# A chunked recurrence: decays counted from a chunk's first token, a first solve level on eight tiles, and one product merged into another block

## The reference

```python
for t in range(S):
    y[:, :, t] = einsum('bhd,bhde->bhe', r_t, state)
    Sa = einsum('bhde,bhe->bhd', state, a_t)
    state = state * w_t[:, :, None, :] - einsum('bhd,bhe->bhde', Sa, b_t) \
            + einsum('bhd,bhe->bhde', v_t, k_t)
```

## Time and profile before

| | us |
|---|---|
| median of the runs | 992.89 |
| the profiled execution | 993.9 |
| its span | 992.2 |
| recurrence, start to the loop's second pass | 0 to 69.1 |
| recurrence, passes 1 to 22 of the loop | 69.1 to 384.4 |
| the two later layers | 384.4 to 992.2 |

### The profile page before, as it was taken

How to read it: one execution, slowest core, us unless ns; L and a number is a source line. 1 busy time by engine, 2 the same in 40 slices (tenths; PEclk the granted TensorE clock), 3 DMA queues, 4 the chain that set the end, 5 groups by cost and what they waited for, 6 DMA issues and landing times.

```text
span 992.2 us, 51897 instructions
## 1 busy us (share of the span) xinstructions
PE 947.2 (95%) x23581; PEld 732.5 (74%) x23582; DVE 465.9 (47%) x964; ACT 270.5 (27%) x503; POOL 275.8 (28%) x297
## 2 busy tenths in 40 slices
PE   4689999999999999999999999999999999999995
PEld 3579989899898996454554554557888888888884
DVE  5447877887887762423143143162352322222220
ACT  1224444444444442201202202202212122122120
POOL 4535566556656651000011010010052101111111
PEclk9789999999999999999999999999999999999999
DMA  5216442333333321780100100047421111001000
GB/s 147 64 50 209 140 123 89 114 104 119 96 115 111 89 72 41 238 271 0 38 27 24 42 28 20 1 133 256 130 88 61 34 34 39 23 28 33 27 29 3
DMA packets 57704, 81.63 MB, mean 82 GB/s; under 512 B 22274, under 2 KB 37454, under 8 KB 57648
## 3 DMA queue, kind: packets, MB, share of 16 engines
q1 hardware_dynamic: 33536, 58.87, 19.0%
q10 hardware_dynamic: 21088, 13.32, 5.2%
q0 software_dynamic: 3024, 8.72, 2.4%
HBM read 68.04 MB, written 14.45 MB: 83 GB/s over the span
## 4 chain that ended last, share of the span: by engine, by line
PE 91%; issue 3%; DVE 2%; DMA 2%; POOL 1%; ACTq 0%; ACT 0%; POOLq 0%; SPq 0%; DVEq 0%
PE ps_D L1478 14%; PE ps_D L224 12%; PE ps_G L1460 6%; PE ps_E L1460 6%; PE ps_B L236 5%; PE ps_E L956 5%; PE ps_B L188 3%; PE ps_G L1467 3%; PE ps_D L1039 3%; PE ps_A L930 3%; PE ps_G L188 3%; PE ps_D L990 2%; PE ps_E L954 2%; PE ps_E L188 2%; PE ps_D L930 2%
## 5 line engine op out<-in xcount | busy, mean ns | idle before, releaser
L1478 PE MATMUL ps_D<-room,hT 128*128 x496 | 139.1, 433 | 0.8 <-issue 0.8
L224 PE MATMUL ps_D<-room 128*128 128x384 f32 x384 | 126.7, 489 | 0.6 <-DVE room L291 0.6
L1478 PEld LDWEIGHTS ps_D<-room,hT 128*128 128x128 f32 x496 | 91.8, 190 | 35.9 <-issue 1.3
L224 PEld LDWEIGHTS ps_D<-room 128*128 128x128 f32 x384 | 72.1, 190 | 51.5 <-issue 1.6
L1421 POOL DMA_INDIRECT out<-y,token x31 | 35.6, 1147 | 258.3 <-DVE y L1585 224.7
L550 POOL DMA_INDIRECT sorted_rows<-rows,slot x24 | 23.9, 997 | 278.3 <-DVE slot L542 272.2
L894 POOL TENSOR_TENSOR room<-room 32x256 f32<-32x256 f32 x96 | 69.5, 724 | 106.5 <-DVE room L1310 101.1
L1521 ACT ACTIVATE hT<-ps_G 128x512 f32<-128x512 f32 x31 | 18.5, 598 | 217.6 <-PE ps_E L1467 211.4
L1585 DVE TENSOR_SCALAR y<-ps_D,x_in 128x320 f32<-128x320 f32 x31 | 17.0, 550 | 125.9 <-PE ps_D L1478 117.5
L1568 DVE COPY w_own<-room 128x1024 f32 x62 | 44.9, 729 | 62.3 <-PE ps_G L1460 33.8
L291 DVE TENSOR_TENSOR room<-ps_D,room 128x384 f32<-128x384 f32 x32 | 17.8, 558 | 113.2 <-PE ps_D L224 107.8
(11 more groups left out here) (225 smaller groups left out, 1646.2 us busy)
## 6 DMA issues: line engine op xcount, KB each, us to landing
room<-in_moe_w SPq DMA_DIRECT2D x8, 1280.0 KB, 12.6
room<-in_moe_w SPq DMA_DIRECT2D x8, 1024.0 KB, 9.2
room<-in_kb SPq DMA_DIRECT2D x48, 160.0 KB
room<-in_vt SPq DMA_DIRECT2D x24, 320.0 KB, 3.1
x_in<-sorted_rows ACTq DMA_DIRECT2D x27, 161.0 KB, 2.3
room<-in_w SPq DMA_DIRECT2D x48, 82.7 KB
room<-in_a SPq DMA_DIRECT2D x48, 80.0 KB
room<-in_r SPq DMA_DIRECT2D x48, 80.0 KB
```

The source lines that it names most:

```text
L224: mm = pe.matmul(self.vs_bank[n % 2][:, 0:TH], self.v[:, s, d * P:(d + 1) * P], self.wspT[:, s, t * TH:(t + 1) * TH], start=(s == 0), stop ...
L1478: mm = pe.matmul(self.ps_y, side.hT[:, u % 2, f, :], self.weights.w2[:, bass.ds(e, 1), f, :], start=(f == 0), stop=(f == self.NF - 1))
```

## The change

It does these things.

- All decays are counted from the first token. The backward scan, `grow`, the copy of the chunk's product and the 16-element reciprocal go. The forward products stay in a ring of four (`decay`), and one reciprocal of all 16 x 32 of them (`inverse`) takes their place; it stands between sum 2 and the mask on `scores_r`, and waits for `kb_start` of the chunk before. GpSimd makes `kb_start` (keys by `inverse`), then `a_start`, then the decayed `state`.
- Level 0 runs on eight tiles with 64 moving columns (the scores and a unit matrix), so that it gives both halves; VectorE adds the unit matrix (`summed(x, 0)`), in place of GpSimd. From there the systems stand on other quarters (`solved`), and the levels write two PSUM banks. `unknowns` runs on eight tiles.
- `own_part` is no block any more. Its 64 matmuls stand alternately with those of level 3, write `ps_A`, and `right_state` adds onto them in PSUM. VectorE's sum for the right-hand side becomes a copy on ScalarE, at the end of its step. Level 3 waits in addition for ScalarE's copy of `turn_kb`.
- `turn_kb` moves ahead of `scores_r`. VectorE's state sum moves ahead of the forward scan. ScalarE's copies of turned data take 40 of 64 columns.

```diff
 # TensorE's loop
-                    own_part(t)
+                    turn_kb(t)
                     scores_r(t)
                     doubling(t, 3)
-                    turn_kb(t)
                     scores_a(t)
 # own part, now inside doubling(t, 3)
+                def until_own(t):
+                    pe.wait_ge(ld_v, t.after16)
+                    pe.wait_ge(kn_d, t.later)
+
+                def own_part(mp, o, n, j):
+                    k = quad(2 * mp + 1 - o)
+                    return pe.matmul(A[solved(mp, o, j), j, n * HD:(n + 1) * HD], xa[k, o, n, j, :], v_tok[k, o, j, n, :],
+                                     start=(n == 0), stop=True, skip_group_check=True)
 # doubling
-                        if l == 1:
-                            pe.wait_ge(init_d, t.after4)
+                        pe.wait_ge(sum_d[l - 1], t.after)
+                        if l == 3:
+                            until_own(t)
...
+                    for n, mp, o, j in by_quad() if l else problems():
+                        q, i = solved(mp, o, j), 4 * j + n
+                        to = q
+                        if l == 0:
+                            q, b = quad(2 * mp + o), 8 * o + 2 * n + j
+                            mm = pe.matmul(levels[to, j, :, n, :], xf[q, o, n, j, :], xa_unit[q, b:GROUPS + 1:GROUPS - b, :],
+                                           start=True, stop=True)
...
+                        if l == 3:
+                            own = own_part(mp, o, n, j)
 # VectorE
                     if is_chunk(x):
                         flip(x, 0)
+                        summed(x, 0)
...
                     if is_chunk(x):
                         flip(x, 1)
                         summed(x, 1)
+                    if is_chunk(c) and c < CHUNKS - 1:
+                        dve.wait_ge(gr_f, c + 1)
+                        dve.wait_ge(state_d, c + 1)
+                        dve.tensor_tensor(grown.rearrange("p m n e -> p n m e"),
...
                     if is_chunk(f):
                         dve.wait_ge(ld_w[f % 2], 32 * (f // 2 + 1))
...
+                        dve.tensor_tensor_scan(decay[:, f % RING, :], w_in[:, f % 2], starts[:, :], 0.0, ALU.mult,
+                                               ALU.add).then_inc(scanned, 1)
...
                     if is_chunk(f):
-                        dve.wait_ge(scan_f, f + 1)
-                        dve.reciprocal(inv_whole[:, :], fwd[:, CH:WCOLS:CH + 1]).then_inc(inv_d, 1)
-                        if f >= 4:
-                            dve.wait_ge(faded_d, f - 3)
-                        dve.tensor_copy(whole[:, f % 4, :], fwd[:, CH:WCOLS:CH + 1]).then_inc(whole_d, 1)
+                        dve.wait_ge(scanned, f + 1)
+                        if f >= 1:
+                            dve.wait_ge(kb_d, f)
+                        dve.reciprocal(inverse[:, :, :], through(f)).then_inc(inv_d, 1)
                     if is_chunk(c):
                         dve.wait_ge(rv_f, c + 1)
                         dve.tensor_tensor(rvu[:, :, :, :], D[:, :, 0:8 * CH].rearrange("p j (m t) -> p j m t", t=CH),
...
-                    if is_chunk(f):
-                        if f >= 1:
-                            dve.wait_ge(kbe_d, f)
-                        dve.tensor_tensor_scan(bwd[:, WCOLS - 1::-1], w_in[:, f % 2, WCOLS - 1::-1],
-                                               starts[:, WCOLS - 1::-1], 0.0, ALU.mult, ALU.add).then_inc(scan_b, 1)
```

More of the change, by code:

```diff
@@ L667 @@
 ROUNDS = 5
+RING = 4
 Counts = namedtuple("Counts", "fixed now after later now2 after4 after16 now32")
@@ L879, in _ @@
                         pool.wait_ge(rh_f, x)
[L880 to L895, removed]
+                        pool.wait_ge(sT_f, x)
@@ L910, in quad, with problems, by_quad, solved @@
                     return slice(q * CH, (q + 1) * CH)
[L912 to L913 removed]
+                def problems():
+                    return [(n, mp, o, j) for n in range(4) for mp in range(2) for o in range(2) for j in range(2)]
+                def by_quad():
+                    return [(n, mp, o, j) for j in range(2) for n in range(4) for mp in range(2) for o in range(2)]
                 def pairs():
                     return [(o, n, mp, j) for o in range(2) for n in range(4) for mp in range(2) for j in range(2)]
+                def solved(mp, o, j):
+                    return quad(2 * (mp ^ j) + o)
                 def right_state(t):
                     pe.wait_ge(as_d, t.after)
[L920 to L921 removed]
+                    pe.wait_ge(state_d, t.after)
                     pe.sem_inc(passed, 1)
[L923 to L925 removed]
+                    for n, mp, o, j in problems():
+                        mm = pe.matmul(A[solved(mp, o, j), j, n * HD:(n + 1) * HD], a_state[rows(j), 4 * o + n, mp, :],
+                                       state[rows(j), 4 * o + n, mp, 0:HD], start=False, stop=True, skip_group_check=True)
                     mm.then_inc(rh_f, 1)
@@ L987, in scores_r @@
                     pe.sem_inc(passed, 1)
-                    for o, n, mp, j in pairs():
-                        m = 4 * o + n
-                        mm = pe.matmul(D[rows(mp), j, m * CH:(m + 1) * CH], vu_d[rows(j), m, mp, :],
-                                       raw_r[rows(j), m, mp, :], start=True, stop=True)
+                    for m, mp, h in [(m, mp, h) for m in range(8) for mp in range(2) for h in range(2)]:
+                        mm = pe.matmul(D[rows(mp), h, m * CH:(m + 1) * CH], vu_d[rows(h), m, mp, :],
+                                       raw_r[rows(h), m, mp, :], start=True, stop=True)
                     mm.then_inc(rv_f, 1)
                 def outputs_state(t):
-                    pe.wait_ge(fT_d, t.now)
+                    pe.wait_ge(sT_d, t.now)
                     pe.wait_ge(ld_rg, t.now32)
@@ L1017, in turn_kb @@
                     else:
-                        pe.wait_ge(state_d, t.now)
-                    turn(A, lambda m: kb_end[:, m].rearrange("p n k t -> p (n k t)"), kT_f)
-                def own_part(t):
-                    pe.wait_ge(ld_v, t.after16)
-                    if not t.fixed or t.now >= 1:
-                        pe.wait_ge(own_d, t.now)
-                    pe.sem_inc(passed, 1)
-                    for j, n, mp, o in blocks():
-                        q, k, i = quad(2 * mp + o), quad(2 * mp + 1 - o), 2 * n + j
-                        mm = pe.matmul(G[q, i * HD:(i + 1) * HD], xa[k, o, n, j, :], v_tok[k, o, n, j, :],
-                                       start=True, stop=True)
-                    mm.then_inc(own_f, 1)
+                        pe.wait_ge(grown_d, t.now)
+                    turn(A, lambda m: kb_start[:, m].rearrange("p n k t -> p (n k t)"), kT_f)
                 def scores_a(t):
-                    pe.wait_ge(ae_d, t.later)
+                    pe.wait_ge(a_d, t.later)
                     if not t.fixed or t.now >= 1:
```

257 lines of the change are left out of this document (119 added, 138 removed).

## The result

The changed kernel takes 1039.07 us (median; 1038.81 to 1039.91), the kernel before 992.89 us. The ratio is 1.0464, with a 95% interval of 1.0446 to 1.0482: slower, by more than the likeliest value of the forecast (1020 us), above the forecast proper (1004 to 1036 us) and inside the stated range (1004 to 1041 us).

A forecast was written before the change was run, and what follows sets the result against it. TensorE was taken as the bound. Twenty passes at +1.37 us (+27.4), two at -0.32 (-0.6) and the prologue (+0.3) gave +27.1 us on 993.9: 1021.0, or 1020 us against the median; forecast 1004 to 1036, range 1004 to 1041.

The forecast's parts named there:

- What bounds, and the new wait: TensorE sets the pace; a 3.4 us reciprocal on VectorE delays the mask, so `scores_a` waits 1.7 us.
- A pass at full clock: Steady loop pass with a reciprocal: 14.01 us of blocks plus 1.7 us wait, 15.7 us, 1.37 more than before.
- the sum: TensorE's blocks in a steady pass, added up if nothing waits: 14.33 us becomes 14.01 us, 0.32 us gained.
- The clock: Rival: TensorE's granted clock falls in the new waits, some ten us or more on top; chance 0.03.
- The rival of more than 8 ns an element: VectorE's new reciprocal takes over 8 ns an element, so the run takes over 1036 us; chance 0.15.
- The pair of reciprocals: VectorE reciprocals of 16 and 6 elements, 255 and 192 ns, both taken as waiting for input: 6.3 ns an element.
- the bounds of 2.0 and 5.1 us: Low and high limits for the 512-element reciprocal on VectorE, from 3.5 and 10 ns an element.
- At no cost: Level 3's wait for ScalarE's copy, GpSimd's order, the keys' product and transfers such as v add no time.
- rival "faster": Reciprocal runs at other operations' rate, under 1.7 us, so TensorE's blocks decide: -7 us, 986 us; chance 0.11.
- Passes 21, 22 and the prologue: Last two passes, without reciprocal: -0.6 us together; prologue and pass 0: +0.3 us, bounds -2 and +4.
- Tiles and banks: Row tiles sharing a PSUM bank do not serialize, by `unknowns` at 10.5 ns a matmul; level 3 1.44 us, otherwise 1.83.
- GpSimd and the scan: Forward scan starts ahead of GpSimd's state product, taking 1.24 us; reversed order, one time in four, 2.18 us, +7 us.

The follow-up runs named there:

- e_copy: Changed kernel with the 512-element reciprocal replaced by a plain copy of the same elements (computation altered); 990.21 us, ratio 0.9968 to the kernel before.
- b_recip: Kernel before the change with an unread reciprocal of 512 forward products added behind its 16-element one; 1062.25 us, ratio 1.0703.
- e_fill6: Changed kernel with six unneeded 128 x 128 matmuls put between level 3 and `scores_a`; 1022.93 us, ratio 1.0306 to the kernel before.
- e_back: Changed kernel with backward scan and 16-element reciprocal put back, GpSimd multiplying them into the inverse; 990.65 us, ratio 0.9977 to the kernel before.

## Why the prediction was right or wrong

- **What bounds, and the new wait: right.** The reciprocal measured 3.33 us (forecast 3.4), the wait before `scores_a` 1.73 us more than between blocks (1.7), put there by the mask on `scores_r` behind it. e_copy and b_recip show that it is the reciprocal.
- **A pass at full clock: 15.53 for 15.7 us.** The blocks without the wait make 15.53 - 1.73 = 13.80, where the sum had 14.01. `unknowns` is 0.69 us to the next start (forecast 0.80, under my lower bound of 0.71): level 1 follows at once. Level 3 with own part is 1.39 us in e_copy, where nothing waits behind it (1.44), level 0 is 0.79 (0.70). The rest lies in blocks of which each was a little shorter than in the row I took for it, such as `scores_r` with 1.06 us for 1.10 and level 2 with 1.03 for 1.06. So the 20 passes cost 24.0 us, not 27.4.
- **The clock: wrong, and this is the step that failed.** The prediction had the fall of the granted clock as a rival with a chance of 0.03, "some ten us or more on top", because TensorE would still be busy for 89% of a pass. It was busy for 13.85 of 15.53 us, 89% indeed, and the clock fell in most passes: 18.9 us of the 44.9. I took the pass's mean for what matters, and put the clock at nothing in the sum. The row of pass 0, with its clock of 0.68 beside 7 us of idle time, was the one to look into. e_fill6 shows the cause by taking the idle time away.
- **That the time fell inside the range is luck.** The forecast proper ended at 1036 us. The range went on to 1041 us for a reciprocal of more than 8 ns an element, and that did not come; the clock, at 0.03, filled its place. Less the clock's 18.9 us the measured time would be near 1020 us, the likeliest value, and that too is partly luck: the passes cost 3.4 us less than forecast, the time ahead of pass 1 2.3 us more and passes 21 and 22 0.6 us more.
- **The rival of more than 8 ns an element: wrong in its cause, though its time (1036 us and over) is what came.** The pair of reciprocals in the earlier trace rows gave 6.3 ns, and 6.26 ns it is. The reason I gave for that pair does not hold, though: the trace of the kernel before also has reciprocals of 6 elements with no recorded wait, and they take 191 to 192 ns, as long as the one that waited.

```profile
L280 DVE RECIPROCAL room<-room x4: 191/191/191, 416.0 to 619.3; 128x6 f32<-128x6 f32 x4
L507 DVE RECIPROCAL esum<-esum x4: 191/192/192, 505.9 to 712.2; 128x6 f32<-128x6 f32 x4
```

  So the agreement is partly luck, and those rows left anything between the bounds of 2.0 and 5.1 us open. The Trainium skill (VectorE: DVE Perf Modes, First, the fixed hardware budget) gives a repeat count of 8 and no time; my estimate from it, 9.4 ns at 1.2 ns an element, is not what this trace shows.
- **At no cost: right with one miss.** The waits for ScalarE's copy and for v do not show. But with `turn_kb` moved I wrote "nothing else is late", and the chain from level 3 over the copy, flip 3 and sum 3 to level 4 is 0.33 us short of cover as soon as the long wait is gone. My rival "faster" at 986 us had the reciprocal's condition right and the time wrong: e_copy takes 990.21 us.
- **Passes 21, 22 and the prologue: mis-sized.** They gave 0.0 for -0.6 us, since the passes without scans were short before as well, 14.19 and 13.95 us; the time ahead of pass 1 grew by 2.6 us for 0.3, inside the bound of 4. e_copy's and e_back's first unknowns come at 43.7 us too, where the kernel before has 42.4, so at least 1.3 us of it is not the long reciprocal. The pass 0 of the changed kernel takes 28.74 us at a mean clock of 0.82, the one before 27.69 at 0.70, and e_fill6, with the same reciprocal, reaches pass 1 1.5 us earlier than the changed kernel. What makes these differences was not tried.
- **Tiles and banks: the row was the better guide.** Level 3 with own part issues 128 loads in 1.31 us, 10.2 ns each, with four row tiles writing one bank of `ps_A`. The Trainium skill (TensorEngine Tiling (Array Packing), Gotcha 1: PSUM Pressure) excludes simultaneous access; the pace shows no cost of that.
- **GpSimd and the scan: the order was right, the price went to GpSimd.** The state product now starts 0.16 us behind the scan and takes 2.17 us for 1.26.

```profile
76.11 2.17 POOL L879 TENSOR_TENSOR room<-room 128x640 f32<-128x640 f32 x1 [0.16 <-DVE room L1266]
```

## What to carry to other kernels

An operation on a busy queue costs what stands behind it: 3.33 us of reciprocal made TensorE wait for 1.7 us a pass in one piece and next to nothing in three. Before replacing two cheap operations by one, find its price per element at sizes near the one you need: two small sizes allowed anything from 3.5 to 10 ns here. Where a change makes TensorE wait, add the clock: here waits of 1.7 us a pass brought 19 us more in 20 passes. And after a move, look again at each pair of blocks that had a dependence hidden by what stood between.

## What the runs showed of the hardware that was not expected

- A reciprocal of float32 takes a time linear in its length: 1134 ns for 160 elements, 1328 for 192, 2332 for 352, 3332 for 512, which is 6.26 ns an element and 0.13 us.
- The granted clock went to its half level with TensorE busy for 89% of a pass and a gap of 1.80 us in each, in 16 passes of 20 and 0.2 to 1.8 us behind the end of the gap; with a gap of 0.79 us it stayed at 1.00, and with six unneeded matmuls in the 1.80 us too.
- VectorE's scan and GpSimd's products hold each other up, whichever comes first: the scan took 2.18 us for 1.24 when a product had started 0.02 us ahead of it, the product 2.17 for 1.26 when the scan had started 0.16 us ahead.
- A 128 x 128 float32 matmul of 128 columns issues two loads: 12 such matmuls made 24 loads in 2.75 us, where 8 transposes of that size take 1.02 us.
